# GpSimd's weight splits moved behind batch 0, and the two heads of a pair side by side in TensorE's scores

## The chip, the cores and the metric

The kernel runs on one core of a Trainium2 chip. The metric is the device time of one execution in microseconds (us). TensorE does the matrix products, VectorE and ScalarE the elementwise work and the copies out of PSUM, GpSimd further elementwise work, and SyncE issues all DMAs.

## The reference

Three stages in a row, all in float32. Stage one is attention on q, k, v of shape (4, 8, 576, 64), in two parts that are added: attention over means of 4 neighbouring positions (144 of them), repeated 4 times, and local attention in which a position sees those less than 4 away.

```
out_d = sm_attn(q_d, k_d, v_d)                 # means of 4 positions
out_up = np.repeat(out_d, factor, axis=2)
mask = np.abs(pos[:, None] - pos[None, :]) < factor
scores = np.where(mask, scale * q @ k^T, -1e9)
attn = softmax(scores); out_local = attn @ v
x = (out_up + out_local) as (2304, 512)
```

Stage two and three are two networks over 2304 tokens:

```
h = x @ w_in; g = h * cos(h); x = g @ w_out                          # d_ff 2048
xn = x / sqrt(mean(x*x) + 1e-6) * rms_g
silu(xn @ w_gate) * (xn @ w_val) @ w_out                             # d_ff 1536
```

## The kernel before, in words

Tokens are cut into six chunks of 384, weights into units of 128 x 512: 32 for the first network, 48 for the second. For each weight the kernel holds a high and a low part, and each product is three matmuls (high with low, low with high, high with high). The high part of a unit is a rounding copy, the low part the difference between the raw weight and the high one. `split_unit` on GpSimd makes them: L423 the high part, L425 the low part. For the first 16 units ScalarE makes the high part (L527), so GpSimd has only L425 to do.

The heads are worked in pairs, four pairs a batch. **Batch 0** (the first four pairs) runs alone, ahead of any network work, with buffers of its own (`Wide`): scores of both heads have their own PSUM banks, and the probability buffers are two deep, so pair j takes those of pair j - 2 (`lag` = 2). **Batches 1 to 3** run beside chunks 0 to 2 of the first network, one batch to a chunk, with one set of buffers (`Narrow`); a table (`PE_WHERE`) says at which of the 19 steps of a chunk TensorE does which step of which pair: step s has the up product of tile s and the down product of tile s - 3. Order is by hand everywhere: each engine's program is a list, in order, and semaphores join them.

One pair goes through: VectorE sums q and k over groups of 4 (L663); TensorE computes the local scores (three mask matmuls L897, L898, L900, ten windows of 64 x 64 at L903) and the downsampled ones (L920), per head; VectorE takes the maximum (L684) and subtracts it into the probability buffer (L690, L691), and the same for the downsampled scores (L697, L699); ScalarE exponentiates (L478, L487); VectorE sums and inverts (L710, L713, L717); GpSimd multiplies (`normalise`, L411 and L414) and, apart from that, sums the values over groups of 4 (`value_sums`, L399 and L404); TensorE transposes (L937, L940), ScalarE and VectorE copy back (L504, L722); TensorE multiplies with the values (L953, L961); ScalarE (L513) and VectorE (L672) add both parts up into XY.

What waits for what around the change, in batch 0: local scores of head u wait until the difference L691 of the head before (`diff_ready`, u - 1) is done; L690 and L691 of pair j wait until the values product of pair j - 2 is done (`pv_done`); the values product of pair j - 2 stands on TensorE behind the scores of the first head of pair j. GpSimd's list is, for each pair, value sums, normalise of head 0, normalise of head 1, then four low parts. In batch 1 it is value sums, two normalises, and 5, 5, 5 and 1 whole units (L423 and L425) behind the four pairs. There the second half of a pair's `value_sums` waits for a DMA that SyncE issues when the first half is done, since both use one buffer. On TensorE, up of tile f waits for unit 2f, down of tile f for unit 2f + 1 (`unit_ready`).

At the entry of chunk 0, ScalarE and VectorE split x into high and low parts (L538, L747), three of four column blocks ahead of the last pair's L672, the fourth behind it.

Of the kernel before, what the change touches and what calls it, by code (L numbers as in the profile page):

```python
# [14 lines left out]
P = 128  # L15
FACTOR = 4
SD = S // FACTOR
# [14 lines left out]
U1, U2 = 2 * F1, 3 * F2  # L32
UP = 4
U_EARLY = UP * PAIRS
BANK = 12
GU = 4
QT = SD // 2


WIN = 64  # L40
REACH = FACTOR - 1
WQ = WIN - 2 * REACH
NW = -(-S // WQ)
TP = NW // 2
Q0 = [WQ * w if w < NW - 1 else S - WIN for w in range(NW)]
K0 = [max(q - REACH, 0) if w < NW - 1 else S - WIN for w, q in enumerate(Q0)]
# [27 lines left out]
def attention_and_two_mlps(nc, qk, vwin, vgrp, w1, w2, rms_g, const, out):  # L74
# [10 lines left out]

    W = [at(f"W{i}", [P, BANK, 2, 512], F32R, slots_at + i * BANK * 4096) for i in range(U2 // BANK)]
    W_raw = [at(f"W_raw{i}", [P, BANK, 2, 512], F32, slots_at + i * BANK * 4096) for i in range(U2 // BANK)]

# [18 lines left out]
    identb = keep("identb", [P, P], BF16)  # L107
    maskb = keep("maskb", [P, 3, WIN], BF16)
# [23 lines left out]
    buffers = {}  # L132
    for i, slot in enumerate((U1, 2 * BANK)):
        part(slots_at + slot * 4096, slots_at + (U2 if i == 0 else U1) * 4096)
# [35 lines left out]
    class Wide:  # L170
# [6 lines left out]
        sl, sd, pt, ptd, pv = SL, SDN, PTP, PTDP, PV  # L177
        qk_in, vw_in, vg_in = ([sem(f"first_{name}_in{j}") for j in range(PAIRS)] for name in ("qk", "vw", "vg"))

    class Narrow:  # L180
# [4 lines left out]
        sl, sd = [X[:, 0:TP * WIN]] * 2, [Z[0:QT, 0:2 * SD]] * 2  # L185
# [13 lines left out]
    qkd_ready = sem("qkd_ready")  # L199
    vt_ready = sem("vt_ready")  # L200
    vd_ready = sem("vd_ready")
    local_scores = sem("local_scores")
    down_scores = sem("down_scores")
    lmax_ready = sem("lmax_ready")
    diff_ready = sem("diff_ready")
# [3 lines left out]
    exp_down = sem("exp_down")  # L209
# [172 lines left out]
    def pool_program(pool):  # L382
# [34 lines left out]
        def split_unit(slot, order, hi_here=True):  # L417

            bank, i = divmod(slot, BANK)
            raw, hi, lo = raw_of(bank, i), part_of(bank, i, 0), part_of(bank, i, 1)  # L420
            hold(pool, group_in[order // GU], 16)
            if hi_here:
                g.tensor_tensor(hi, raw, ones[:, 0:1].to_broadcast([P, 512]), ALU.mult).then_inc(unit_hi, 1)  # L423
            hold(pool, unit_hi, order + 1)
            g.tensor_tensor(lo, raw, hi.bitcast(F32), ALU.subtract).then_inc(unit_ready, 1)  # L425
            hold(pool, unit_ready, order + 1)


        for j in range(PAIRS):
            value_sums(Wide, 0, j)  # L430
            normalise(Wide, 0, j, 0)
            normalise(Wide, 0, j, 1)
            for u in range(UP * j, UP * j + UP):
                split_unit(u, u, hi_here=False)

        def batch(b, units=(0,) * PAIRS):

            first = U_EARLY
            for j in range(PAIRS):
                value_sums(Narrow, b, j)  # L440
                normalise(Narrow, b, j, 0)
                normalise(Narrow, b, j, 1)
                for u in range(first, first + units[j]):
                    split_unit(u, u)
                first += units[j]
            scale_y(b - 1)

# [9 lines left out]
                g.tensor_tensor(y_tile(c, t), y_tile(c, t), rinv[:, t:t + 1].to_broadcast([P, 512]), ALU.mult).then_inc(y_scaled, 1)  # L457


        batch(1, (5, 5, 5, 1))  # L460
        with pool.Fori(2, B) as b:
            batch(b)
        for u in range(GU):
# [415 lines left out]
    def pe_program(pe):  # L879
        t_ = nc.tensor  # L880
# [42 lines left out]
        def scores(kind, b, j, s):  # L923
            local(kind, b, j, s)
            downsampled(kind, b, j, s)
# [17 lines left out]
        def values(kind, b, j):  # L943
# [19 lines left out]
                                    pt[64 * r:64 * r + 64, c0:c0 + COUNT[w]], start=True, stop=True)  # L963
            ins.then_inc(pv_done, 1)

        pe.wait_ge(setup_dve, 3)
        pe.wait_ge(zeroed, 3)
        for j in range(PAIRS):
            scores(Wide, 0, j, 0)
            if j >= 2:  # L970
                values(Wide, 0, j - 2)
            if j >= 1:
                transposes(Wide, 0, j - 1, 0)
            scores(Wide, 0, j, 1)
            if j >= 1:
                transposes(Wide, 0, j - 1, 1)
        values(Wide, 0, PAIRS - 2)
        transposes(Wide, 0, PAIRS - 1, 0)
# [175 lines left out]
```

## Time and profile before

| | |
|---|---|
| median of 3 runs | 1022.74 us |
| lowest, highest | 1019.49, 1027.27 us |
| profiled execution, span from first to last instruction | 1022.4 us |
| batch 0 (until the first product of chunk 0 runs through) | about 60 us |
| chunk 0 with batch 1 | about 60 to 159 us |

The profile is of one execution; no time of that execution other than its span is given. Of the engines PE is TensorE's matmuls, PEld its weight loads, DVE VectorE, ACT ScalarE, POOL GpSimd, SPq SyncE's queue. A row of a timeline has start, duration, engine, line, operation, what is written and read, shapes, and how many instructions are merged in it; in brackets stands the idle time ahead and what ended it. A float32 matmul leaves two records, so the ten windows of one head are 20.

### The profile page before, as it was taken

To read this page: it belongs to the slowest core of one execution; us is meant where nothing else is said; L and a number is where in the kernel's file an instruction comes from. 1 tells how busy PE (TensorE), PEld (TensorE's weight loads), DVE (VectorE), ACT (ScalarE), POOL (GpSimd) and SP (SyncE) were. 2 spreads that over 40 slices of the span, in tenths; PEclk is the share of its full clock that TensorE was granted. 3 is DMA by queue.
4 is the path that set the end of the run, shared out by engine and by line. 5 is a ranking of instruction groups with operands and counts; after the bars stand their busy time and mean duration, and the time that the engine had idled before them with its cause. 6 is when DMAs were issued, how large, how long until landed. Compare 5 with 4: busy or idle time off the path is not lost.

```text
span 1022.4 us, 17445 instructions
## 1 busy us (share of the span) xinstructions
PE 991.5 (97%) x6320; PEld 887.3 (87%) x6320; DVE 516.8 (51%) x1176; ACT 426.6 (42%) x923; POOL 259.8 (25%) x285
## 2 busy tenths in 40 slices
PE   6889999999899999999999999999999999999998
PEld 5677787888788899998997999999999999999997
DVE  6767776676676664554667424324324324324322
ACT  3556566665665665655655213113113113112111
POOL 4947763221422150100299930000000000000000
PEclk9999999999999999999999999999999999999999
DMA  9622111111111100000134000000000000000000
GB/s 275 210 92 92 52 51 54 51 51 52 52 51 51 63 2 1 1 0 0 42 124 135 31 1 1 31 0 0 31 0 0 31 0 0 31 0 0 31 1 31
DMA packets 19208, 43.95 MB, mean 43 GB/s; under 512 B 1616, under 2 KB 1744, under 8 KB 19152
## 3 DMA queue, kind: packets, MB, share of 16 engines
q1 hardware_dynamic: 19152, 43.16, 12.9%
q8 instruction: 40, 0.66, 0.3%
q14 instruction: 16, 0.13, 0.0%
HBM read 38.44 MB, written 4.72 MB: 42 GB/s over the span
## 4 chain that ended last, share of the span: by engine, by line
PE 82%; DVE 6%; ACT 4%; POOL 3%; issue 3%; DMA 1%; DVEq 0%; SPq 0%; POOLq 0%; ACTq 0%
PE ps L984 26%; PE ps L986 25%; PE ps L985 25%; PE ps L903 2%; POOL W L425 1%; DVE ub L781 1%; ACT ub L576 1%; PE ps L920 1%; PE ps L1065 1%; DVE ub L779 1%; ACT ub L578 1%; DMA qk<-qk 1%; DVE XY L672 1%; ACT probd L487 1%; PE ps L937 1%
## 5 line engine op out<-in xcount | busy, mean ns | idle before, releaser
L984 PE MATMUL ps<-xs,W 128*128 128x384 f32 x960 | 327.8, 341 | 1.9 <-DVE xs L747 1.4
L986 PE MATMUL ps<-xs,W 128*128 128x384 f32 x960 | 324.0, 338 | 4.1 <-issue 4.1
L985 PE MATMUL ps<-xs,W 128*128 128x384 f32 x960 | 323.4, 337 | 0.0
L984 PE MATMUL ps<-W,ring 128*128 128x512 f32 x504 | 202.8, 402 | 0.0
L986 PE MATMUL ps<-W,ring 128*128 128x512 f32 x504 | 199.1, 395 | 0.0
L985 PE MATMUL ps<-W,ring 128*128 128x512 f32 x504 | 198.7, 394 | 0.0
L984 PEld LDWEIGHTS ps<-xs,W 128*128 128x128 f32 x960 | 181.4, 189 | 15.6 <-issue 7.6
L985 PEld LDWEIGHTS ps<-xs,W 128*128 128x128 f32 x960 | 181.6, 189 | 4.6
L986 PEld LDWEIGHTS ps<-xs,W 128*128 128x128 f32 x960 | 181.4, 189 | 0.0
L839 DVE TENSOR_TENSOR ub<-ub,ps 128x384 f32<-128x384 f32 x72 | 39.9, 554 | 248.9 <-ACT ub L629 248.9
L629 ACT ACTIVATE ub<-ps 128x384 f32<-128x384 f32 x72 | 35.4, 492 | 270.0 <-PE ps L986 270.0
L986 PEld LDWEIGHTS ps<-W,ring 128*128 128x128 f32 x504 | 94.9, 188 | 20.9
L984 PEld LDWEIGHTS ps<-W,ring 128*128 128x128 f32 x504 | 95.1, 189 | 18.6 <-issue 2.7
L985 PEld LDWEIGHTS ps<-W,ring 128*128 128x128 f32 x504 | 95.2, 189 | 15.8
L425 POOL TENSOR_TENSOR W<-W_raw,W 128x512 fp32r<-128x512 f32 x68 | 91.4, 1343 | 5.3
L787 DVE TENSOR_TENSOR ub<-ub,ps 128x384 f32<-128x384 f32 x96 | 53.0, 552 | 70.2 <-ACT ub L578 70.2
L570 ACT ACTIVATE ub<-ps,consts 128x384 f32<-128x384 f32 x96 | 55.1, 574 | 56.0 <-PE ps L986 54.2
L576 ACT ACTIVATE ub<-ub 128x384 f32<-128x384 f32 x96 | 50.4, 525 | 65.7 <-DVE ub L781 65.7
L635 ACT ACTIVATE ring<-ub 128x384 fp32r<-128x384 f32 x72 | 37.8, 525 | 82.6 <-DVE ub L843 82.6
L779 DVE TENSOR_SCALAR ub<-ub 128x384 f32<-128x384 f32 x96 | 44.7, 466 | 50.5 <-ACT ub L570 50.4
L848 DVE TENSOR_TENSOR ring<-ub,ring 128x384 fp32r<-128x384 f32 x72 | 42.7, 594 | 39.6 <-ACT ring L635 39.6
L751 DVE TENSOR_TENSOR ring<-ub,ring 128x384 fp32r<-128x384 f32 x96 | 60.9, 634 | 2.5 <-ACT ring L547 2.5
(91 smaller groups left out, 1014.5 us busy)
## 6 DMA issues: line engine op xcount, KB each, us to landing
W_raw<-w SPq DMA_DIRECT2D x17, 1024.0 KB, 6.1
qk<-qk SPq DMA_DIRECT2D x14, 576.0 KB, 4.1
vw<-vwin SPq DMA_DIRECT2D x14, 384.0 KB, 3.1
out<-XY SPq DMA_DIRECT2D x18, 256.0 KB, 2.0
vg<-vgrp SPq DMA_DIRECT2D x26, 144.0 KB
qk_more<-qk SPq DMA_DIRECT2D x2, 576.0 KB, 16.1
vg_more<-vgrp SPq DMA_DIRECT2D x6, 144.0 KB
vw_more<-vwin SPq DMA_DIRECT2D x2, 384.0 KB, 15.5
```

What stands on the lines that cost most here:

```text
L425: g.tensor_tensor(lo, raw, hi.bitcast(F32), ALU.subtract).then_inc(unit_ready, 1)
L570: a.activation(v, HB[f % NH], ACT.Identity, scale=INV_2PI, bias=consts[:, 0:1]).then_inc(turns_ready, 1)
L576: a.activation(v, v, ACT.Abs).then_inc(abs_ready, 1)
L635: a.activation(ring[:, f % 3, 0, :], ub[:, f % 2, :], ACT.Copy).then_inc(ahi_ready, 1)
L751: v.tensor_tensor(ring[:, f % 3, 1, :], ub[:, f % 2, :], ring[:, f % 3, 0, :].bitcast(F32), ALU.subtract).then_inc(glo_ready, 1)
L779: v.tensor_scalar(w, w, MAGIC, -2.0 * math.pi, ALU.subtract, ALU.mult).then_inc(angle0, 1)
L787: v.tensor_tensor(w, w, HB[f % NH], ALU.mult).then_inc(g_done, 1)
L839: v.tensor_tensor(w, w, GB[f % 2], ALU.mult).then_inc(silu_ready, 1)
L848: v.tensor_tensor(ring[:, f % 3, 1, :], w, ring[:, f % 3, 0, :].bitcast(F32), ALU.subtract).then_inc(alo_ready, 1)
L984: t_.matmul(dst, a_lo, b_hi, start=first, stop=False, skip_group_check=True)
L985: t_.matmul(dst, a_hi, b_lo, start=False, stop=False, skip_group_check=True)
L986: return t_.matmul(dst, a_hi, b_hi, start=False, stop=last, skip_group_check=True)
```

## The change

On GpSimd, the low parts of units in batch 0 leave the loop over pairs and stand behind it, and are 10 instead of 16. The other six come in batch 1, whose counts of units behind the four pairs go from 5, 5, 5, 1 to 8, 8, 6, 0; units 10 to 15 have only the low part to do there. On TensorE, in batch 0 alone, the scores of both heads of a pair are written as one block in which the heads alternate matmul by matmul. The block waits for the differences of both heads of the pair before, and signals both heads at its end.

```diff
+U_FIRST = 10
...
             normalise(Wide, 0, j, 0)
             normalise(Wide, 0, j, 1)
-            for u in range(UP * j, UP * j + UP):
-                split_unit(u, u, hi_here=False)
+        for u in range(U_FIRST):
+            split_unit(u, u, hi_here=False)
...
-            first = U_EARLY
+            first = U_FIRST
...
-                    split_unit(u, u)
+                    split_unit(u, u, hi_here=u >= U_EARLY)
...
-        batch(1, (5, 5, 5, 1))
+        batch(1, (8, 8, 6, 0))
...
+        def both_local(j):
+            if j:
+                pe.wait_ge(diff_ready, 2 * j)
+            pe.wait_ge(Wide.qk_in[j], 16)
+            for s in range(2):
+                sl = Wide.sl[s]
...
+            for w in range(NW):
+                half, t = w % 2, w // 2
+                for s in range(2):
+                    q, k = (Wide.qk[j][64 * s:64 * s + 64, a, :] for a in range(2))
+                    ins = t_.matmul(Wide.sl[s][64 * half:64 * half + 64, t * WIN:t * WIN + WIN], q[:, Q0[w]:Q0[w] + WIN], k[:, K0[w]:K0[w] + WIN],
+                                    start=False, stop=w >= NW - 2, skip_group_check=True)
+            ins.then_inc(local_scores, 2)
+
+        def both_downsampled(j):
+            pe.wait_ge(qkd_ready, j + 1)
+            if j:
+                pe.wait_ge(exp_down, 2 * j)
+            for t in range(2):
+                for s in range(2):
+                    q, k = (Wide.qkd[j][64 * s:64 * s + 64, a, :] for a in range(2))
+                    ins = t_.matmul(Wide.sd[s][:, t * SD:t * SD + SD], q[:, t * QT:t * QT + QT], k, start=True, stop=True)
+            ins.then_inc(down_scores, 2)
...
         for j in range(PAIRS):
-            scores(Wide, 0, j, 0)
+            both_local(j)
+            both_downsampled(j)
             if j >= 2:
                 values(Wide, 0, j - 2)
             if j >= 1:
                 transposes(Wide, 0, j - 1, 0)
-            scores(Wide, 0, j, 1)
-            if j >= 1:
                 transposes(Wide, 0, j - 1, 1)
```

Line numbers shift: by one up to GpSimd's and TensorE's code (L425 becomes L426), and the new blocks are L974 to L977 (masks), L982 (windows) and L994 (downsampled).

On GpSimd in batch 0, between the normalises of the second pair (prob_89) and those of the third (prob_81), before:

```order
L414 TENSOR_TENSOR probd_90<-probd_90,recip 72x288
L425 TENSOR_TENSOR W_49<-W_raw_52,W_49 128x512 x4
L399 TENSOR_TENSOR vg_more_97<-vg_more_97 72x2x128
L404 TENSOR_TENSOR vd_more_93<-vg_more_97 72x2x64
L399 TENSOR_TENSOR vg_more_98<-vg_more_98 72x2x128
L404 TENSOR_TENSOR vd_more_93<-vg_more_98 72x2x64
L411 TENSOR_TENSOR prob_81<-prob_81,recip 128x320
```

And at the end of batch 0 of the change, where batch 1 follows with vg_79:

```order
L412 TENSOR_TENSOR prob_89<-prob_89,recip 128x320
L415 TENSOR_TENSOR probd_90<-probd_90,recip 72x288
L426 TENSOR_TENSOR W_49<-W_raw_52,W_49 128x512 x10
L400 TENSOR_TENSOR vg_79<-vg_79 72x2x128
L405 TENSOR_TENSOR vd_80<-vg_79 72x2x64
```

The four low parts behind a pair are gone from between the pairs; ten stand behind the last.

On TensorE in batch 0, the second pair (qk_85, qkd_91) with the transposes of the first, before:

```order
L897 MATMUL ps<-maskb,identb 128x64
L898 MATMUL ps<-maskb,identb 128x192
L900 MATMUL ps<-maskb,identb 128x64
L903 MATMUL ps<-qk_85 64x64 x10
L920 MATMUL ps<-qkd_91 72x144 x2
L937 MATMUL ps<-ident,prob_81 128x128 x3
L940 MATMUL ps<-ident,probd_82 72x72 x4
L897 MATMUL ps<-maskb,identb 128x64
L898 MATMUL ps<-maskb,identb 128x192
L900 MATMUL ps<-maskb,identb 128x64
L903 MATMUL ps<-qk_85 64x64 x10
L920 MATMUL ps<-qkd_91 72x144 x2
```

And now:

```order
L977 MATMUL ps<-maskb,identb 128x64
L974 MATMUL ps<-maskb,identb 128x64
L975 MATMUL ps<-maskb,identb 128x192
L977 MATMUL ps<-maskb,identb 128x64
L982 MATMUL ps<-qk_85 64x64 x20
L994 MATMUL ps<-qkd_91 72x144 x4
L938 MATMUL ps<-ident,prob_81 128x128 x3
L941 MATMUL ps<-ident,probd_82 72x72 x4
L938 MATMUL ps<-ident,prob_81 128x128 x3
L941 MATMUL ps<-ident,probd_82 72x72 x4
```

The second head's scores have moved ahead of the first transposes, and the 20 windows stand in one run.

## Rows read from the trace of the kernel before

**Rows 1.** The page: busy time, share of the span and instructions of each engine

```profile
PE 991.5 (97%) x6320; PEld 887.3 (87%) x6320; DVE 516.8 (51%) x1176; ACT 426.6 (42%) x923; POOL 259.8 (25%) x285
```

**Rows 2.** Windows: stretch, length, busy us (instructions) per engine, granted clock, DMA

```profile
10.00:15.00 5.00, 5.00 (x52) 4.01 (x51) 4.38 (x12) 2.83 (x8) 2.30 (x4) 1.00 1.04 347
```

**Rows 3.** Timeline of GpSimd, batch 0: start, duration, what

```profile
28.89 5.30 POOL L425 TENSOR_TENSOR W<-W_raw,W 128x512 fp32r<-128x512 f32 x4
...
35.60 0.72 POOL L399 TENSOR_TENSOR vg_more<-vg_more 72x256 f32<-72x256 f32 x1
...
38.48 0.72 POOL L411 TENSOR_TENSOR prob<-prob,recip 128x320 f32<-128x320 f32 x1
```

**Rows 4.** Timeline of VectorE in batch 0

```profile
9.13 0.43 DVE L691 TENSOR_TENSOR prob<-ps,lmax 128x320 f32<-128x320 f32 x1
...
12.68 0.17 DVE L713 TENSOR_SCALAR sums<-sums 128x7 f32<-128x7 f32 x1
...
27.37 0.11 DVE L690 MEMSET prob<- 128x64 f32 x1 [1.54 <-PE ps L961]
...
28.24 0.59 DVE L699 TENSOR_SCALAR dbias<-dmax 72x2 f32<-72x2 f32 x1
...
31.93 0.95 DVE L713 TENSOR_SCALAR sums<-sums 128x7 f32<-128x7 f32 x1
...
33.56 0.11 DVE L690 MEMSET prob<- 128x64 f32 x1
...
38.48 0.11 DVE L690 MEMSET prob<- 128x64 f32 x1 [1.53 <-PE ps L961]
```

**Rows 5.** Timeline of TensorE in batch 0, and one L903 row of chunk 0

```profile
9.57 0.24 PE L897 MATMUL ps<-maskb,identb 128*128 128x64 bf16 x1
...
9.95 1.33 PE L903 MATMUL ps<-qk 64*64 64x64 f32 x20
11.22 1.23 PE L920 MATMUL ps<-qkd 64*72 64x144 f32 x4
...
24.52 1.23 PE L953 MATMUL ps<-probd,vd 72*64 72x144 f32 x8
25.68 1.53 PE L961 MATMUL ps<-prob,vw 64*64 64x58 f32 x40
...
63.27 0.80 PE L903 MATMUL ps<-qk 64*64 64x64 f32 x20
```

**Rows 6.** Timeline, all engines, from batch 0 into chunk 0

```profile
51.13 5.49 POOL L425 TENSOR_TENSOR W<-W_raw,W 128x512 fp32r<-128x512 f32 x4
...
53.54 1.23 PE L953 MATMUL ps<-probd,vd_more 72*64 72x144 f32 x8 [0.59 <-ACT prob L504]
53.91 4.13 DVE L747 TENSOR_TENSOR xs<-XY,xs 128x384 fp32r<-128x384 f32 x3 [0.46 <-ACT xs L538]
...
59.69 0.56 DVE L747 TENSOR_TENSOR xs<-XY,xs 128x384 fp32r<-128x384 f32 x1 [0.59 <-ACT xs L538]
...
60.30 0.45 PE L984 MATMUL ps<-xs,W 128*128 128x384 f32 x1 [1.41 <-DVE xs L747]
```

**Rows 7.** Timeline of GpSimd beside chunk 0, splits of the second pair and after

```profile
100.25 1.04 POOL L423 TENSOR_TENSOR W<-W_raw,ones 128x512 fp32r<-128x512 f32 x1
...
113.05 0.73 POOL L399 TENSOR_TENSOR vg<-vg 72x256 f32<-72x256 f32 x1
...
117.30 0.73 POOL L399 TENSOR_TENSOR vg<-vg 72x256 f32<-72x256 f32 x1 [2.60 <-DMA vg<-vgrp]
...
124.42 1.04 POOL L423 TENSOR_TENSOR W<-W_raw,ones 128x512 fp32r<-128x512 f32 x1
```

**Rows 8.** Timeline of TensorE in chunk 0, places of the transposes

```profile
126.62 0.49 PE L937 MATMUL ps<-ident,prob 128*128 128x128 f32 x3
...
147.79 0.49 PE L937 MATMUL ps<-ident,prob 128*128 128x128 f32 x3
```

**Rows 9.** Windows of chunk 0, columns as in Rows 2

```profile
90.00:92.00 2.00, 2.00 (x8) 1.96 (x7) 1.41 (x6) 1.18 (x4) 0.31 (x1) 0.50 0.29 74
```

More of the change, by code:

```diff
@@ L964, in values @@
             ins.then_inc(pv_done, 1)
+        def both_local(j):
[4 more added lines that the diff above has]
+                sl = Wide.sl[s]
+                t_.matmul(sl[:, 0:WIN], identb[:, :], maskb[:, 0, :], start=True, stop=False, skip_group_check=True)
+                t_.matmul(sl[:, WIN:(TP - 1) * WIN].rearrange("p (t k) -> p t k", k=WIN), identb[:, :],
+                          maskb[:, 1:2, :].to_broadcast([P, TP - 2, WIN]), start=False, stop=False, skip_group_check=True)
+                t_.matmul(sl[:, (TP - 1) * WIN:TP * WIN], identb[:, :], maskb[:, 2, :], start=False, stop=False, skip_group_check=True)
+            for w in range(NW):
[14 more added lines that the diff above has]
+            ins.then_inc(down_scores, 2)
         pe.wait_ge(setup_dve, 3)
```

## The prediction

> **What bounds the kernel now.** I read the page's engine line first: TensorE is busy for 97% of the span, GpSimd for 25% [rows 1]. So from chunk 0 on, whatever keeps TensorE from starting lengthens the kernel one for one, and the only stretch where something else can be the bound is the one ahead of it, batch 0. The granted clock of TensorE says 1.00 there [rows 2], but the same 20 records of L903 take 1.33 us in batch 0 and 0.80 in chunk 0 [rows 5]: in batch 0 TensorE works at the lower of its two rates, 1.2 GHz, and its column for the clock must not be believed so early.
>
> Then the timelines of batch 0. GpSimd spends 5.30 us on four low parts behind each pair [rows 3], and the chain of waits of that stretch runs over GpSimd alone. This invites the reading that three such blocks, 15.9 us, come off. What has to be asked is what is late next. VectorE shows it: L690, the first instruction that writes the probabilities of a new pair, waits at 27.37 and at 38.48 for TensorE's values product, not for GpSimd [rows 4]. The turn between the two is 11.11 us. Counted on TensorE alone, a pair is two heads of scores, each 0.38 (masks) + 1.27 (windows) + 1.2 (L920) = 2.8, two lots of transposes of about 1.15, and values of 2.85 (24.52 to 27.37): 10.8 us [rows 4, 5]. So TensorE's order is as long as GpSimd's; taking GpSimd's blocks away alone would give at most 0.3 us a turn. That is why the change's other half matters.
>
> **Part one, the interleaved scores.** What TensorE saves: L961 puts 40 records through in 1.53 us where L903 needs 1.33 for 20 [rows 5]. Both are products of 64 rows by 64 columns; L961 uses both row halves of the array in turn, L903 of one head stays in one half. With the heads alternating L903 becomes like L961. The two heads' windows then take between 1.2 us (as L961, start to start) and 2.54 (no overlap, twice 1.27); I take 1.2, since L961 is the same form in the same stretch. L920, whose two heads also use different halves, takes between 1.2 and 2.4; I take 1.2 for the same reason. Six masks: 0.6 to 0.76, I take 0.6.
>
> What it costs: the block waits for the differences of **both** heads of the pair before, where the first head used to wait for one. That closes a new ring, per turn:
> - VectorE from L690 of head 0 to L690 of head 1: 33.56 - 27.37 = 6.19. In it L713 takes 0.95 and L699 0.59, where L713 takes 0.17 when GpSimd is idle [rows 4]; both are held by GpSimd's work, so without it 6.19 - 0.78 - 0.42 = 4.99.
> - L691 to TensorE's mask: 9.13 to 9.57, with 0.03 ahead of it, 0.47 [rows 4, 5].
> - Masks 0.6, windows 1.2, L920 1.2.
> - Values of two pairs before, until L690: 2.85.
>
> Sum 11.3 us, against 11.11. TensorE is relieved by 2.7 us a turn and stands idle for it; the turn does not get shorter. The third pair's L690 comes about 0.6 us later than before (its values product stands behind a block of 3.0 us that waits for the second difference), the fourth pair's 0.8 later. In the tail the order helps: no further scores wait, L713 and L699 are short, and the last normalise no longer stands behind four low parts. Walking the same durations from there, the last values product starts at 52.8 instead of 53.54 [rows 6]: **-0.7 us**. Bounds: +6 if nothing overlaps on TensorE, -3 if VectorE's part is 1 us shorter in each turn than I count.
>
> **Part two, ten low parts behind batch 0.** GpSimd now reaches them at about 48.6 and needs 10 x 1.34 = 13.4 us [rows 3], until about 62. Before, 4 of them ran from 51.13 to 56.6; in that time VectorE's three L747 took 4.13 us, 1.38 each, and the fourth, with GpSimd idle, 0.56 at 59.69 [rows 6]. The first three stay slow. The fourth now meets GpSimd as well, and TensorE waits for exactly it (1.41 us idle at 60.30 [rows 6]): **+0.8 us**, between 0 and 1.3. The Trainium skill (SBUF — State Buffer, section "SBUF: two separate sides") says that VectorE with two SBUF inputs and GpSimd take a shared port pair as an exclusive lock, and the loser waits out the whole instruction; by it alone the fourth L747 would wait up to one low part, 1.27 us, and the sum would be 0.4 higher. Entry into chunk 0 is therefore where it was, within 0.1 us: the whole of batch 0 is worth nothing. The ten units last until tile 4; units 10 to 15 follow behind the first pair of batch 1 at about 77 to 84, and tile 5 is started at 79, tile 6 at 88, so no product waits for a weight.
>
> **Part three, 8, 8, 6, 0.** Behind the first pair nothing moves: six low parts and two whole units cost 13.5 us, five whole units cost 12.8, and GpSimd waits over 1 us for VectorE right after. Behind the second pair, five units took 113.05 - 100.25 = 12.8, 2.56 each [rows 7]. Eight take 20.5, so the third pair's value sums start at 120.7 instead of 113.05. Their second half starts 4.25 later (the buffer is single: 117.30 - 113.05 [rows 7]), and from there to the end of the first head's normalise is 2.88 (35.60 to 38.48 [rows 3]): 127.7 with the shortest transfer. TensorE wants to transpose at 126.62 [rows 8]: **+1.1 us**. The splits behind the third pair begin at 129.5 instead of 124.42 [rows 7]; six take 15.4, to 144.9; with 4.1 and 2.88 the fourth pair's first normalise ends at 151.7 (151.4 to 152.0). TensorE wants it at 147.79 + 1.1 = 148.9 [rows 8]: **+2.8 us**. Nothing gives these back, since TensorE runs the rest of chunk 0 without idle time and nothing stands ahead of the transposes that could be taken first. SyncE's queue moves with GpSimd: values and next q, k stand behind the second half of vg, some 5 to 8 us later than before, and are still in time.
>
> **Sum.** -0.7 + 0.8 + 1.1 + 2.8 = +4.0 us. Against the profiled span of 1022.4 that is 1026.4; the median of the runs, 1022.74, lies 0.3 above that span, so I forecast **1026.8 us**. A measurement of this kernel tells about 1%, 10 us, from no change (its runs spread from 1019.49 to 1027.27).
>
> **Rivals.**
> - **A, forecast (0.45)**, with a variant (0.12) in which the stall of 2.8 us also lets the clock fall. The clock was 0.50 at 90 to 92 [rows 9], behind a wait of TensorE for VectorE's L672. Such a fall costs about 1.7 us (3.4 us at half rate): 1028.5.
> - **B, slower: the heads don't overlap on TensorE (0.06).** The masks, the different PSUM banks or the queue keep them in a row. Then the block is 5.6 us, a turn 11.3 + 2.5 = 13.8, and two blocks more of this length lie in the start; some 6 to 7 us on top, 1033. It decides as soon as 20 windows take over 1.5 us. Against it: L961.
> - **C, batch 0 does get shorter (0.14).** If the ring is not closed as I count it (VectorE's share smaller, work of L663 and L672 off it), the turn falls to VectorE's own 8.6 to 9 us, 2.3 less over some three turns: -7 + 4.7, about 1020.5. The full 15.9 us of GpSimd's blocks (1010) would need both other engines to follow, which their rows exclude (0.03).
> - **D, the clock (0.07).** Denser products in batch 0 might lift TensorE to 2.4 GHz before 58 us. In the stretch of 10 to 15 us it was busy for 5.00 of 5.00 us [rows 2] and the rate stayed low, which speaks against it. At the full rate the ring is 11.3 - 2.4 = 8.9, with shorter last transposes -6 in all: 1021. The Trainium skill (TensorE: Matmul & The Clock Gate, section "The HAM clock gate") says that sustained activity releases the lower rate; by it the higher rate should long have been there, and this trace doesn't bear it out.
> - **E, the stalls in chunk 0 are smaller (0.13)**: second halves land earlier or TensorE comes later; 1023 to 1024.
>
> **The numbers.** Of these, the cases from 1020 to 1029 hold 0.9. The range reaches below to C with a part of the runs' spread and above to B: **1017 to 1032**. Faster by over 1% (under 1012.5) needs most of GpSimd's blocks to come off: 0.04. Slower by over 1% (over 1033) needs B with the stalls: 0.06. Within 1%: 0.90.
>
> **What would show it.** Right: in batch 0 of the changed kernel TensorE has idle time ahead of the masks, ended by L691, and the distance of waiting L690s is 11 to 11.6; L982's 40 records take about 1.5 us; the fourth L747 is over 1 us; TensorE waits at the transposes of the third and fourth pair for GpSimd's L415, by about 1 and 3 us. Wrong: first product of chunk 0 running through before 58 us; no wait at those transposes; L982 over 2 us.

## The result and the profile after

The changed kernel takes **1027.58 us** in the median of 20 runs (1025.76 to 1030.43). The kernel before, run beside it, takes 1023.92 us (1018.96 to 1029.64, 20 runs). The ratio is 1.0042, with a 95% interval of [1.0029, 1.0054]: slower by 4.3 us by the ratio (3.7 us between the two medians), well under the 1% that was set as the bound for "no change", and clear of zero. Forecast were 1026.8 us and +4.0 us.

The profiled execution has a span of 1027.8 us. The page, answering to [rows 1]:

```profile
PE 985.6 (96%) x6320; PEld 881.7 (86%) x6320; DVE 514.7 (50%) x1176; ACT 426.9 (42%) x923; POOL 259.3 (25%) x285
```

TensorE has the same 6320 matmuls and is 5.9 us less busy in a span that is 5.4 us longer. The lines of the source stand one later than before up to the scores (L690 is now L691, L747 is L748, L414 is L415), and the three lines of a product are L1014 to L1016.

TensorE in batch 0, answering to [rows 5] (start, duration, engine, line, operation, tiles, shape, number of instructions merged, idle time ahead and what ended it):

```profile
5.44 0.21 PE L974 MATMUL ps<-maskb,identb 128*128 128x64 bf16 x1 [5.44 <-DMA qk<-qk]
...
12.54 0.24 PE L974 MATMUL ps<-maskb,identb 128*128 128x64 bf16 x1 [3.97 <-DVE prob L692]
...
31.29 0.23 PE L974 MATMUL ps<-maskb,identb 128*128 128x64 bf16 x1 [0.28 <-DVE prob L692]
...
31.94 1.35 PE L982 MATMUL ps<-qk_more 64*64 64x64 f32 x40
33.21 1.24 PE L994 MATMUL ps<-qkd 64*72 64x144 f32 x8
34.38 1.23 PE L954 MATMUL ps<-probd,vd 72*64 72x144 f32 x8
35.54 1.53 PE L962 MATMUL ps<-prob,vw 64*64 64x58 f32 x40
```

VectorE in the same stretch, answering to [rows 4]:

```profile
25.79 0.11 DVE L691 MEMSET prob<- 128x64 f32 x1 [3.29 <-PE ps L962]
...
26.66 0.17 DVE L700 TENSOR_SCALAR dbias<-dmax 72x2 f32<-72x2 f32 x1
...
29.94 0.17 DVE L714 TENSOR_SCALAR sums<-sums 128x7 f32<-128x7 f32 x1
...
30.78 0.11 DVE L691 MEMSET prob<- 128x64 f32 x1
...
37.23 0.11 DVE L691 MEMSET prob<- 128x64 f32 x1 [3.39 <-PE ps L962]
```

Read the two together and the ring of the prediction stands there term by term: L691 to L691 of one pair 30.78 - 25.79 = 4.99, L691 to the mask 0.51, masks 0.65, windows of both heads 1.27, downsampled scores 1.17, values 2.85 (34.38 to 37.23). Sum and distance of the waiting L691s are 11.44 us; before it was 11.11 [rows 4].

All engines from batch 0 into chunk 0, answering to [rows 6]:

```profile
46.38 14.20 POOL L426 TENSOR_TENSOR W<-W_raw,W 128x512 fp32r<-128x512 f32 x10
...
50.43 1.23 PE L954 MATMUL ps<-probd,vd_more 72*64 72x144 f32 x8 [0.59 <-ACT prob L505]
50.81 4.38 DVE L748 TENSOR_TENSOR xs<-XY,xs 128x384 fp32r<-128x384 f32 x3 [0.46 <-ACT xs L539]
...
56.83 1.25 DVE L748 TENSOR_TENSOR xs<-XY,xs 128x384 fp32r<-128x384 f32 x1 [0.59 <-ACT xs L539]
...
58.14 0.69 PE L1014 MATMUL ps<-xs,W 128*128 128x384 f32 x1 [1.57 <-DVE xs L748]
...
60.86 0.52 PE L1016 MATMUL ps<-xs,W 128*128 128x384 f32 x1
61.18 0.47 PE L1014 MATMUL ps<-xs,W 128*128 128x384 f32 x1
61.49 0.34 PE L1015 MATMUL ps<-xs,W 128*128 128x384 f32 x1
...
62.62 0.80 PE L904 MATMUL ps<-qk 64*64 64x64 f32 x20
```

The low parts run from 46.38 to 60.6, and the fourth L748 takes 1.25 us where it took 0.56 [rows 6]. Behind it the products come 0.32 us apart until 61.2 and 0.17 apart from 61.5: TensorE entered the chunk at its lower rate. In the kernel before, the rate had risen inside the first three blocks of products, ahead of the wait:

```profile
57.60 0.51 PE L985 MATMUL ps<-xs,W 128*128 128x384 f32 x1
57.92 0.36 PE L986 MATMUL ps<-xs,W 128*128 128x384 f32 x1
```

GpSimd and TensorE later in chunk 0 of the changed kernel, answering to [rows 7] and [rows 8], one fence for each:

```profile
120.28 0.74 POOL L400 TENSOR_TENSOR vg<-vg 72x256 f32<-72x256 f32 x1
...
124.06 0.73 POOL L400 TENSOR_TENSOR vg<-vg 72x256 f32<-72x256 f32 x1 [2.50 <-DMA vg<-vgrp]
...
128.49 1.24 POOL L424 TENSOR_TENSOR W<-W_raw,ones 128x512 fp32r<-128x512 f32 x1
...
144.03 0.74 POOL L400 TENSOR_TENSOR vg<-vg 72x256 f32<-72x256 f32 x1
...
147.74 0.73 POOL L400 TENSOR_TENSOR vg<-vg 72x256 f32<-72x256 f32 x1 [2.44 <-DMA vg<-vgrp]
```

```profile
127.00 0.54 PE L938 MATMUL ps<-ident,prob 128*128 128x128 f32 x3 [0.62 <-POOL probd L415]
...
150.68 0.54 PE L938 MATMUL ps<-ident,prob 128*128 128x128 f32 x3 [2.28 <-POOL probd L415]
```

The value sums of the third pair start at 120.28 (forecast 120.7), the splits behind it at 128.49 (129.5), and both waits of TensorE are there.

**Where the 4 us are.** In the profile before the first mask matmul stood at 6.80, after it at 5.44, because the first q and k landed earlier (4.8 to 5.4 in every other profile of this study), so I count from the first mask:

| from the first mask, us | before | after | difference |
|---|---|---|---|
| last values product of batch 0 | 46.74 | 44.99 | -1.75 |
| first product behind the fourth L747/L748 | 53.50 | 52.70 | -0.80 |
| L903/L904 of the first pair in chunk 0 | 56.47 | 57.18 | +0.71 |
| end of chunk 0 (GpSimd's scale of y) | 154.90 | 159.00 | +4.10 |

The last row is GpSimd's first instruction behind the chunk, of before and of after:

```profile
161.70 0.20 POOL L451 TENSOR_SCALAR msq<-ssq 128x3 f32<-128x3 f32 x1 [11.28 <-ACT ub L596]
```

```profile
164.44 0.20 POOL L452 TENSOR_SCALAR msq<-ssq 128x3 f32<-128x3 f32 x1 [12.35 <-ACT ub L597]
```

In these two profiles, of one execution each, a loss as large as that of the medians stands there at the end of chunk 0. In both the clock falls twice in chunk 0 (88.7 and 112.6 before, 88.8 and 112.7 after), so the falls do not enter this difference.

### The profile page after: what moved, and what is told of

It reads as the page before. It is cut to its first block, busy times and chain, and to the rows that moved or that the text cites. A ratio compares the mean times of both kernels' runs of the same rounds, so it can differ in the third digit from the quotient of the medians.

```text
span 1027.8 us, 17445 instructions
## 1 busy us (share of the span) xinstructions
PE 985.6 (96%) x6320; PEld 881.7 (86%) x6320; DVE 514.7 (50%) x1176; ACT 426.9 (42%) x923; POOL 259.3 (25%) x285
## 4 chain that ended last, share of the span: by engine, by line
PE 80%; DVE 7%; POOL 4%; ACT 4%; issue 3%; DMA 1%; DVEq 0%; ACTq 0%; POOLq 0%; SPq 0%
PE ps L1014 25%; PE ps L1016 24%; PE ps L1015 24%; POOL W L426 2%; POOL W L424 1%; PE ps L904 1%; DVE ub L782 1%; ACT ub L577 1%; DVE XY L673 1%; PE ps L1095 1%; PE ps L921 1%; PE ps L962 1%; ACT ub L579 1%; DVE ub L780 1%; ACT probd L488 1%
## 5 line engine op out<-in xcount | busy, mean ns | idle before, releaser
L1014 PE MATMUL ps<-xs,W 128*128 128x384 f32 x960 | 328.4, 342 | 2.1 <-DVE xs L748 1.6
L1016 PE MATMUL ps<-xs,W 128*128 128x384 f32 x960 | 324.9, 338 | 4.1 <-issue 4.1
L1014 PE MATMUL ps<-W,ring 128*128 128x512 f32 x504 | 203.0, 403 | 0.0
L1016 PE MATMUL ps<-W,ring 128*128 128x512 f32 x504 | 199.9, 397 | 0.0
L1014 PEld LDWEIGHTS ps<-xs,W 128*128 128x128 f32 x960 | 182.0, 190 | 16.3 <-issue 7.7
L1016 PEld LDWEIGHTS ps<-xs,W 128*128 128x128 f32 x960 | 181.9, 189 | 0.0
L1016 PEld LDWEIGHTS ps<-W,ring 128*128 128x128 f32 x504 | 95.1, 189 | 21.0
L1014 PEld LDWEIGHTS ps<-W,ring 128*128 128x128 f32 x504 | 95.3, 189 | 18.5 <-issue 2.7
L426 POOL TENSOR_TENSOR W<-W_raw,W 128x512 fp32r<-128x512 f32 x68 | 92.1, 1354 | 5.3
```

What stands on the lines that cost most here:

```text
L1014: t_.matmul(dst, a_lo, b_hi, start=first, stop=False, skip_group_check=True)
L1016: return t_.matmul(dst, a_hi, b_hi, start=False, stop=last, skip_group_check=True)
```

## The experiments

Each is the changed kernel with the edit shown, unless it says otherwise, timed against the kernel before on the same chip. Profiles are of one execution each. The question was first whether the two halves of the change act as I said, and then why removing the stalls did not show in the median.

**1. The splits alone**, TensorE's order as before.

```diff
-            both_local(j)
-            both_downsampled(j)
+            scores(Wide, 0, j, 0)
...
+            scores(Wide, 0, j, 1)
```

> Only GpSimd's part of the change; TensorE's scores in the order of before. Theory (the slowdown is GpSimd's later normalises in chunk 0; the paired scores give batch 0 nothing): TensorE still waits about 0.6 and 2.3 us for GpSimd at the transposes of the third and fourth pair, batch 0 from the first mask to the last values product is 44 to 46 us (changed kernel 45.9, before 47.9), ratio to before 1.002 to 1.005. Rival (the paired scores are what lets batch 0 keep up once GpSimd is out of the way): batch 0 back to 47.5 us or more, 1.5 us slower than the changed kernel, ratio 1.005 to 1.007.

1028.91 us, ratio 1.0044 [1.0026, 1.0062]. The waiting L691s stand at 24.07 and 34.84, 10.77 apart (counted for the prediction: 10.8), and batch 0 is 43.34 long from the first mask, 1.65 **shorter** than in the profile with the interleaved heads (how much of that is the order is taken up under run 7). The two waits at the transposes are 1.02 and 2.51 us. With run 2 beside it, the loss comes from this half.

**2. The heads alone**: `U_FIRST` 16 inside the loop over pairs, and units 5, 5, 5, 1, as before.

> Only TensorE's part of the change; GpSimd's order and counts (16 low parts in batch 0; 5, 5, 5, 1) as before. Theory: no waits for GpSimd at the transposes of chunk 0, batch 0 within 0.5 us of 47.9 since GpSimd's low parts stand in its chain again, ratio 0.999 to 1.001. Rival (the wait for both heads is what costs): batch 0 longer by 1 us or more, ratio over 1.002.

1023.48 us, 1.0009 [0.9992, 1.0026]: no difference. The turn is 11.46 (27.78 to 39.24), no wait for L415, and the fourth L748 takes 0.56 again. Batch 0 is 48.21 long, 1.5 longer than before, which the expectation had as a sign of the rival; the ratio over 1.002 that was to come with it did not. Most of the 1.5 is gone at the entry, where the first three L748 take 3.10 us against 4.13: the first product behind the fourth stands at 53.95 from the first mask, before at 53.50.

**3. Fourteen low parts behind batch 0**, so that six units stand behind the second pair:

```diff
-U_FIRST = 10
+U_FIRST = 14
...
-        batch(1, (8, 8, 6, 0))
+        batch(1, (6, 6, 6, 0))
```

> The changed kernel with 14 low parts behind batch 0 and 6, 6, 6, 0 units in batch 1 (instead of 10 and 8, 8, 6, 0). GpSimd is idle for 8 us between 62 and 72 us, so four more low parts fit. Theory: the waits of TensorE at the transposes of the third and fourth pair (0.6 and 2.3 us) go, chunk 0 ends 2.9 us earlier against the entry than in the changed kernel, ratio to before 0.999 to 1.002. Rival (TensorE's waits there are made up elsewhere, or the loss lies in the lower clock at the entry): ratio stays at 1.004.

1027.04 us, 1.0042 [1.0026, 1.0058]. The trace does what the edit says: one wait of 0.41 us is left at the transposes, in place of 0.62 and 2.28. The time does not: 0.999 to 1.002 was expected. The stalls were real and their removal did not show in the median (1.0030 in a second measurement, run 9), which is what the later runs had to explain.

**4. The same block with one head behind the other** (the loop over windows inside the loop over heads; the downsampled scores in the same way).

```diff
-            for w in range(NW):
-                half, t = w % 2, w // 2
-                for s in range(2):
+            for s in range(2):
+                for w in range(NW):
+                    half, t = w % 2, w // 2
```

> The changed kernel with the same block and the same waits, but in it the ten windows of head 0 and then those of head 1, and the downsampled scores likewise: no alternation. Theory (two row halves of the array run side by side only when the heads alternate): L982's 40 records take 2.6 us instead of 1.35, L994's 8 take 2.4 instead of 1.24, the block is 2.4 us longer, four times in batch 0, which becomes 8 to 10 us longer; ratio to before 1.012 to 1.014. Rival (order inside the block does not matter): L982 at 1.35 us, ratio 1.004.

1031.96 us (6 runs), 1.0076 [1.0049, 1.0103]. Its TensorE in batch 0:

```profile
33.54 2.04 PE L982 MATMUL ps<-qk_more 64*64 64x64 f32 x40
35.51 1.24 PE L994 MATMUL ps<-qkd 64*72 64x144 f32 x8
```

Start to start the 40 records of the windows take 1.97 us against 1.27 when the heads alternate, and the turn is 12.14 against 11.44, longer by just these 0.70. So alternating does put two heads side by side. The effect is less than a third of what was expected (2.6 us for L982, 2.4 for L994, a ratio from 1.012): the windows of one head behind the other still take less than twice the 1.27 of one head [rows 5], and L994 takes 1.17 start to start in either order. TensorE's time is on the ring here, which it would not be if the ring were VectorE's alone (rival C).

**5. The low parts left out.** In place of the first ten low parts GpSimd writes zeros, so the products with these ten units lack their low terms:

```diff
+            if order < U_FIRST:
+                g.memset(lo.bitcast(F32), 0.0).then_inc(unit_ready, 1)
```

> The changed kernel, but for the first ten units GpSimd writes zeros instead of the low part (the low parts of ten weight units are left out of the computation): GpSimd is free soon after batch 0. Theory (GpSimd's run of ten beside the entry into chunk 0 slows VectorE there): the first three L748 take 0.6 instead of 1.46 us each, the fourth 0.55 instead of 1.25; from the last values product of batch 0 to the fourth L748 2 us or more is saved, and the stretch from there to the scores of the second pair is nearer the 26.5 us of before than the 28.2 of the changed kernel. The waits at the transposes (0.6 and 2.3) stay. Ratio to before 1.000 to 1.002. Rival (the lower clock at the entry alone costs, GpSimd does not): the stretch stays at 28, ratio 1.003 to 1.005.

1024.68 us against 1023.11, 1.0007 [0.9989, 1.0025]. Entry of that kernel:

```profile
48.63 1.50 DVE L751 TENSOR_TENSOR xs<-XY,xs 128x384 fp32r<-128x384 f32 x3 [0.46 <-ACT xs L542]
...
53.05 0.56 DVE L751 TENSOR_TENSOR xs<-XY,xs 128x384 fp32r<-128x384 f32 x1 [0.59 <-ACT xs L542]
```

Three x splits take 1.50 us in place of 4.38 and the fourth 0.56 in place of 1.25, while the waits at the transposes stay (0.62 and 2.47). So it is GpSimd's low parts that slow VectorE at the entry. The ratio is 0.0035 lower than the changed kernel's, with both stalls still there. That is more than what moving the low parts costs: four of them stood beside the first three x splits before too (4.13 us), and this run is rid of those as well. In its profile TensorE's rate is also high from 53.9, where it was low until 61.2 in the changed one; from the last values product to L904 (here L907) it takes 8.50 us against 12.19, and 9.73 before.

**6. TensorE kept busy at the entry.** 21 extra matmuls, 128 x 128 in bfloat16, whose result nobody reads, stand between the last transposes and values of batch 0 and behind them:

```diff
+        def fill(n):
+            for _ in range(n):
+                t_.matmul(ps[:, 2, 0:P], identb[:, :], identb[:, :], start=True, stop=True, skip_group_check=True)
...
+        fill(5)
         transposes(Wide, 0, PAIRS - 1, 1)
+        fill(4)
         values(Wide, 0, PAIRS - 1)
+        fill(12)
```

> The changed kernel with 21 matmuls of 128 x 128 whose result nothing reads, put where TensorE waits at the end of batch 0 (5 ahead of the last transposes, 4 ahead of the last values product, 12 behind it), 107 ns each at the lower rate. Theory (TensorE's rate at the entry is what its idle time before made it; the changed kernel ran its first up products at 0.32 us a matmul until 61.5, before it was 0.17 from 58): the higher rate comes earlier and the first steps take 1 to 1.5 us less, ratio 1.002 to 1.004. Rival (when the rate rises is independent of such fillers): time unchanged, 1.004 to 1.006.

1024.62 us, 1.0012 [0.9994, 1.0031]: 0.0030, some 3 us, below the changed kernel, more than the 1.002 to 1.004 expected. I took that for a proof that the rate at the entry was the loss, and it is not one. TensorE reaches the higher rate at 57.4 instead of 61.5, and the stretch from the first product behind the fourth L748 to L904 is 2.98 us instead of 4.48. Against it stand a batch 0 that is 1.13 us longer (46.12 against 44.99), all of it ahead of the first filling, where VectorE waits 0.32 and 0.78 us for q and k, and stalls at the two transposes of 2.49 and 1.43, which is 1.0 more together. At the end of chunk 0, counted from the first mask, the kernel is 0.64 us ahead of the changed one (158.36 against 159.00), with one fall of the clock fewer in that chunk. Most of the gain comes later, and run 12 shows from what.

**7. Fourteen units with the old order of the heads.**

> Scores in the order of before, GpSimd as in the run with 14 low parts and 6, 6, 6, 0 units. Theory: batch 0 as in the run with the splits alone (43.3 us from first mask to last values product, before 46.7), no wait for GpSimd at the transposes; but the 3.4 us won go at the entry, since GpSimd's low parts lie beside the first steps of chunk 0. Ratio 0.999 to 1.002. Rival (the extra low parts beside the first steps cost as much as the waits did, as the run with 14 and paired heads suggests with 1.0042): 1.003 to 1.005.

1023.94 us, 1.0019 [1.0002, 1.0036], one wait of 0.43 us at the transposes. Run 3, with the paired block, was at 1.0042 on another chip; the intervals overlap, so the order of the heads is not shown to cost time. Nor does the length of batch 0 show it, as it differs between profiles with the same instructions there: up to the last values product it is 42.95 (runs 3 and 5), 44.16 (run 10), 44.64 (run 9), 44.99 (the changed kernel) and 46.12 (run 6) with the paired block, and 43.34 (run 1), 43.53 (this run) and 45.19 (run 11) with the old order. What the order does change is the turn: where TensorE stays at its lower rate, it is 11.44 and 11.46 with the block, 10.77, 10.69 and 10.80 without. Run 3 has only 10.30, because the values product in the turn fell into a stretch at the higher rate (1.71 us in place of 2.85):

```profile
33.31 0.71 PE L954 MATMUL ps<-probd,vd 72*64 72x144 f32 x8
33.95 0.91 PE L962 MATMUL ps<-prob,vw 64*64 64x58 f32 x40
```

**8. Three edits to open the ring**: fourteen units, values of two pairs before between the local and the downsampled scores, and VectorE's differences of both heads together.

```diff
             both_local(j)
+            if j >= 2:
+                values(Wide, 0, j - 2)
             both_downsampled(j)
...
-            less_max(Wide, 0, j, 0)
+            less_local_max(Wide, 0, j, 0)
+            less_local_max(Wide, 0, j, 1)
```

> Paired heads and 14 low parts (6, 6, 6, 0), and two edits in batch 0: TensorE does the values product of pair j - 2 between the local and the downsampled scores of pair j, and VectorE does the differences of both heads one behind the other, ahead of its other work on the pair. Theory (the ring of batch 0 is both differences, the block, the values product): distance between the waiting L691 of the third and fourth pair falls from 11.44 to 10.6 or less, last values product 1.5 to 2 us earlier than with 14 alone (42.95). Ratio 0.999 to 1.003. Rival (another ring of the same length stands behind): distance stays over 11.2, ratio as with 14 alone, 1.004.

1026.57 us, 1.0028 [1.0006, 1.0049]. The turn is 11.17, shorter than the changed kernel's by 0.27 only, where 10.6 or less was expected; the rival's bound of 11.2 was not met either. The time lies in the theory's range without the mechanism that it was to follow from.

**9 to 11. Fourteen units again, and with the fillings in both orders of the heads.**

> The same kernel as fourteen, for a second profile and a second ratio. If the clock is the reason why the removed waits do not show (falls of the granted clock that come more often), the second profile shows at least three falls of 3.4 us by the end of the first transition and a ratio of 1.002 to 1.005 again. If the first ratio was a matter of chance, it is 1.000 to 1.002, since batch 0 is about 3.8 us shorter and the waits of 2.9 us are gone.

> The change with 14 units ahead (splits behind the pairs 6, 6, 6, 0) and 21 filling products of 128x128 ahead of the last transposes and values of batch 0. If both measured losses are separate and add (the waits of 0.6 and 2.3 us at L415, gone with fourteen units; the lower rate at the entry into chunk 0, gone with the filling), the ratio is 1.0042 - 0.0030 (what the filling gave, 1.0042 to 1.0012) - 0.0028 (2.9 us) = 0.9984, some 1021.5 us. If fourteen units give nothing in the median for a reason that the filling doesn't touch, as fourteen alone (1.0042), it is 1.0012, like filled_entry. If the three low parts more beside the entry eat what the filling gives, 1.004.

> The same with the scores of batch 0 head by head as in the kernel before. If the filling is worth 0.0030 here too: 1.0019 - 0.0030 = 0.9989, some 1022 us; if the filling does nothing where batch 0 is short, 1.002.

Measured on one chip against 1024.16 us for the kernel before: fourteen again 1026.28 us, 1.0030 [1.0013, 1.0048]; filled 1021.22 us, 0.9980 [0.9965, 0.9995]; filled with the old order of the heads 1021.02 us, 0.9981 [0.9965, 0.9996]. The granted clock of the second profile of fourteen units, by windows (stretch, length, busy us (instructions) per engine, granted clock, DMA):

```profile
160.00:166.00 6.00, 5.07 (x20) 4.96 (x20) 3.60 (x5) 2.79 (x6) 5.05 (x7) 0.72 0.02 4
259.00:265.00 6.00, 4.59 (x18) 4.48 (x18) 3.94 (x5) 3.22 (x7) 4.01 (x5) 0.72 0.01 3
556.00:562.00 6.00, 5.43 (x21) 4.43 (x22) 3.07 (x10) 1.78 (x7) 5.61 (x6) 0.72 0.40 151
```

It has five falls of 3.4 us (86.6, 110.5, 161.7, 260.7, 557.6), the profile before three (88.7, 112.6, 259.3). Over the 35 runs of the kernel before that stand beside runs 5 to 8, a run's time goes with its time at low clock at 0.40 us for each us, so by an estimate such a fall costs about 1.4 us, and two more of them would take back what the removed stalls gave. This rests on single profiles: the first profile of fourteen units (run 3) has four falls, at 57.5, 159.9, 258.9 and 555.8. At the end of chunk 0, where fourteen again has two falls like the kernel before and the changed one, it stands at 155.46 from the first mask, against 154.90 and 159.00, so the cure does act there; chunk 1, with the fall at 161.7, then takes 99.87 us against 97.52. And not all of the stalls comes back in chunk 0: TensorE's other waits in it are 5.0 us in fourteen again and 3.4 before (at L921/L920 for ScalarE alone 0.89 against 0.24). In the two profiles with fillings and fourteen units none comes at 160 or 260; of the one with the old order of the heads:

```profile
157.00:163.00 6.00, 6.00 (x54) 5.48 (x53) 5.58 (x9) 3.61 (x9) 4.51 (x6) 1.00 0.00 1
255.00:261.00 6.00, 6.00 (x55) 5.22 (x54) 5.55 (x11) 3.65 (x7) 4.91 (x6) 1.00 0.00 0
```

What stands ahead of the falls at 160 and 260 is a wait of TensorE that nothing in the profile ends ("issue"). In the kernel before:

```profile
161.80 0.34 PE L986 MATMUL ps<-xs,W 128*128 128x384 f32 x1 [2.08 <-issue]
...
259.30 0.47 PE L986 MATMUL ps<-xs,W 128*128 128x384 f32 x1 [1.98 <-issue]
```

In the changed one:

```profile
164.47 0.33 PE L1016 MATMUL ps<-xs,W 128*128 128x384 f32 x1 [2.02 <-issue]
...
262.38 0.34 PE L1016 MATMUL ps<-xs,W 128*128 128x384 f32 x1 [2.07 <-issue]
```

They stand at the start of chunks 1 and 2, and chunks 0 to 2 are one loop on TensorE (`pe.Fori(0, ACH)`), so they are the second and third pass. No profile with the fillings has them.

**12. The fillings alone in the kernel before**, nothing of the change.

> The kernel before with the 21 filling products alone, nothing of the change. The filling gave 0.0030 to 0.0050 in three kernels with the changed splits. If it works on the clock whatever the splits are, this kernel comes to 0.996 (some 1020 us) and nothing of the change is needed for the gain of 0.998. If the filling only repairs what the later splits do to the entry, it is 0.999 to 1.001 here, since the entry of the kernel before has the higher rate from 57.96 already. A third outcome, 1.002, would mean that the fillings stand in the way here, because TensorE waits for less time in this tail.

1021.58 us against 1023.25, **0.9976** [0.9965, 0.9988]: between the 0.996 and the 0.999 of the first two cases expected, and clearly faster, although this kernel's entry had the higher rate already. Its page has this row of DMA queues:

```profile
q8 instruction: 22, 0.36, 0.1%
```

where the kernel before, and the changed one, have

```profile
q8 instruction: 40, 0.66, 0.3%
```

and for the stretch of 175 to 360 us alone, passes two and three of the loop, 1 packet with the fillings and 15 without:

```profile
q8 instruction: 1, 0.02, 0.0%
```

```profile
q8 instruction: 15, 0.25, 0.6%
```

(packets, MB, share of the DMA engines.) The ten profiles of this study without fillings all have 40 packets and both waits (1.76 to 2.48 us), the four with them 22 packets and no such wait; the wait that ends at 161.80 before has the one packet of 159 to 162 us at its start. I read it so: with 21 more matmuls ahead of it, the loop over chunks is not fetched again on each pass; without them it is, and its second and third pass then start with a wait of 2 us. The two waits and what follows are visible in the ends of chunks 0, 1 and 2 of this kernel:

```profile
160.05 0.20 POOL L451 TENSOR_SCALAR msq<-ssq 128x3 f32<-128x3 f32 x1 [11.29 <-ACT ub L596]
256.99 0.20 POOL L451 TENSOR_SCALAR msq<-ssq 128x3 f32<-128x3 f32 x1 [13.82 <-ACT ub L596]
353.60 0.20 POOL L451 TENSOR_SCALAR msq<-ssq 128x3 f32<-128x3 f32 x1 [13.82 <-ACT ub L596]
```

96.94 and 96.61 us, where the kernel before has 97.52 and 99.01 (161.70, 259.22, 358.23), the second with the fall at 259.3 in it. The filled one has a fall of its own in the first of them, at 172.3, and four in all. Not the whole 4.1 us of the waits are won, because TensorE then comes earlier to another wait, 10 us into the pass:

```profile
170.59 0.71 PE L920 MATMUL ps<-qkd 64*72 64x144 f32 x4 [1.70 <-ACT probd L487]
```

against 0.24 us there before; the fall at 172.3 comes right behind it. The Trainium skill (Runtime: NRT & Kernel Launch, section "Instruction fetch mechanics") says that a taken branch to code that is no longer held makes the sequencer fetch it by DMA before it goes on; by that rule the wait belongs to the loop's jump back, and the trace agrees in the place and in the packets, 15 against 1. That it is the position of the loop in the code and not something else of the fillings was not tried with instructions that take no time.

## Why the prediction was right

**The ring in batch 0** (turn 11.3, measured 11.44 and 11.46): right, each term within 0.07 us. That the heads overlap was the assumption behind it; runs 1 and 4 show both, the overlap (1.27 against 1.97 us) and that TensorE's relief brings nothing to the turn (10.77 without the block). It is the ring at TensorE's lower rate: runs 3, 5, 9 and 10 have the same instructions and turns of 10.30 to 10.80, with a values product wholly or partly at the higher rate in them.

**Batch 0, -0.7 us**: measured -1.75, in the bounds of +6 to -3. Up to the first waiting L690/L691 it is -0.22, the turn +0.33, and the tail from the last waiting one to the last values -1.86, where I counted -1.5. Two things I had not priced: the third pair's waiting L691 comes 0.22 earlier and the fourth's 0.11 later, where I gave them 0.6 and 0.8 later, and in the profile before the values product of the third pair starts at 46.60, as GpSimd's L404 for it ends (46.19 + 0.45); it stood behind four low parts. That wait is put down to "issue" there, and I had missed it. With 42.95 to 46.12 us for the same instructions (run 7), the -1.75 is one draw out of a spread of 3 us, and that it lies near the -0.7 says little.

**The fourth L747, +0.8 us**: it takes 1.25 against 0.56, +0.69; with the three ahead of it (4.38 against 4.13) the entry costs +0.95 (from -1.75 to -0.80). Run 5 shows the cause: with GpSimd's low parts gone it is 0.56. The rule of the Trainium skill (SBUF — State Buffer, section "SBUF: two separate sides") on the shared port pair would have allowed a wait of up to one low part, 1.27 as I had it. The trace does not contradict the lock (1.25 is 0.69 longer than 0.56, and a low part takes about 1.35), but no run here tells a lock from two engines that slow each other, and the +0.8 was nearer than the full wait.

**TensorE's rate at the entry**: missing from the sum. From the first product behind the wait to L904 it is 4.48 us after and 2.97 before, +1.51, nearly all of it in the ten products at 0.32 us spacing. I had taken the rate of the profile before, high from 57.92, as given. The change is not shown to be what lowered it: two profiles of one and the same kernel have 4.33 (run 3) and 2.96 us (run 9) there. Rival D had the clock of batch 0 only as a gain. In fact both happened in the changed kernel: the clock was high for a short stretch in batch 0, and low again until the chunk had begun.

```profile
17.20:20.40 3.20, 1.09 (x13) 0.91 (x13) 3.04 (x9) 1.27 (x4) 2.56 (x5) 1.00 1.05 396
20.60:61.40 40.80, 30.90 (x355) 25.21 (x356) 26.30 (x81) 19.62 (x53) 26.00 (x30) 0.50 0.43 151
```

The short stretch holds little work of TensorE (1.09 us of 3.20); on the ring it shortens one set of masks, 0.39 us (20.08 to 20.47) in place of 0.65. In run 3 such stretches give 2.2 us, over two values products.

**The stalls, +1.1 and +2.8 us**: 0.62 and 2.28, with 1.02 and 2.51 in run 1, 0.62 and 2.47 in run 5. Place, engine and cause are right; both are about 0.5 too large. One term of mine was too long in both: the second half of the value sums starts 3.78 and 3.71 us behind the first, and I had 4.25 and 4.1. In this trace, which starts 1.36 earlier, GpSimd had the last L415 of the head done 0.8 and 1.2 ahead of the counted 127.7 and 151.7, and TensorE wanted it 0.2 and 0.5 ahead of the counted 126.6 and 148.9. Runs 3 and 7 take them away, but for 0.41 and 0.43, by the count of units alone. That they are worth their 2.9 us in the median is not shown: run 3, without them, measured no faster than the changed kernel, and run 9 by 0.0012.

**The sum** of +4.0 meets the measured +4.10 at the end of chunk 0, but not by itself: -1.05 (batch 0) and -1.0 (stalls) against +0.15 (fourth L747) and +1.5 (rate at the entry), and +0.5 in pieces under 0.35 us. I count the stalls, the ring and the slow fourth L748 as shown. The closeness of the total is luck in good part: it needed the +1.5 of the rate at the entry, which I had not foreseen and which differs between profiles of one kernel, to stand against a batch 0 and stalls that were each a whole microsecond off. Of the spans' 5.4 us, 2.7 are there at 161.70/164.44, with the later start of the profile before; the rest lies in single executions' falls of the clock, of which the changed kernel has one more, at 559.8.

**The rivals.** B (no overlap) is out by the changed kernel itself, whose 40 records take 1.27 us start to start; run 4 shows what they take without alternation. C (batch 0 shorter) is half true of the splits alone: batch 0 gets 3.4 us shorter there (43.34 against 46.74), and all of it is lost again until the second pair's scores, 79.94 us from the first mask against 80.03. The variant of A, in which the clock falls behind the 2.8 us stall, did not occur: the profile of the changed kernel has no fall between 116 and 262 us.

**What stays open.** Which part of the median's 4 us the stalls are, since they go in run 3 and the time stays, and stay in run 5 and the time goes. Whether fourteen units have more falls of the clock than the kernel before, as their two profiles have it, and why. The number varies from run to run with one and the same program (time 1023.34 to 1029.65 in twelve runs of fourteen again), and no run here sets it by hand.

## What to carry to other kernels

Taking work off the engine that bounds a prologue brings what the next ring allows, and the removed work still has to be done: ask beside which instructions it now stands. Before explaining a few microseconds by the edit, look at the waits that nothing ends and at the instruction packets of the DMA queues: a loop whose code is fetched again on every pass costs 2 us a pass here, and an edit ahead of it can switch that off, as 21 matmuls did. Then test the suspected cure on the unchanged kernel too: the fillings in the kernel before gave the lowest ratio of this study (0.9976), and with the change beside them it was no better (0.9980, 0.9981). And before a difference of 1 or 2 us between two profiles is put down to an edit, take a second profile of the same kernel: here two of them differ by 1.7 us in batch 0 alone (42.95 and 44.64).

## What the runs showed of the hardware that I had not expected

- The code of a loop can cost or not cost: 40 instruction packets and two waits of 2.0 to 2.1 us before and after, or 22 packets and none with 21 extra matmuls outside the loop. By where it lies, I believe; this was not tried apart.
- The alternation of row halves works across two heads with different PSUM banks: the 40 records (20 products) of 64 x 64 take 1.27 us start to start at the lower rate, the 20 records of one head 1.27 as well [rows 5]. Even one head behind the other, 40 take 1.97 and not 2.5.
- The granted clock of a stretch is only good once a change of it has been recorded: for 50 to 62 us the view of the kernel before says 1.00 while its products come 0.32 us apart until 57.9; that of the changed kernel, which has a change at 17.1, says 0.52 for the same stretch.

```profile
50.00:62.00 12.00, 9.35 (x81) 7.72 (x80) 8.98 (x23) 5.06 (x10) 8.64 (x10) 1.00 0.19 64
```

```profile
50.00:62.00 12.00, 10.00 (x70) 8.61 (x71) 9.52 (x17) 5.04 (x11) 11.20 (x10) 0.52 0.01 2
```
